# A fifth chunk of q and k split by GpSimd, in the place of the first, with TensorE's order to match

## The reference

```
qn = q / (norm(q, axis=tokens) + 1e-6)      kn = k / (norm(k, axis=tokens) + 1e-6)
a  = softmax(kn.T @ qn / tau)               # 256 x 256
x  = v @ a                                  # 6016 x 256
h  = x @ w_in1;  x = (max(h, 0) ** 2) @ w_out1
h  = x @ w_in2;  y = max(0.01 * h, h) @ w_out2
```

## Time and profile before

| | us |
|---|---|
| median of 3 runs | 1022.01 (1021.99 to 1022.23) |
| the profiled run | 1026.41 |
| span of its records | 1024.6 |
| TensorE busy in the span | 1018.3 (99%) |
| VectorE, ScalarE, GpSimd busy | 726.7, 673.4, 26.4 |
| granted TensorE clock, from 0 to 75 us | 1.00 in each 5 us |

### The profile page before, as it was taken

How to read it: one execution, slowest core, us unless ns; L and a number is a source line. 1 busy time by engine, 2 the same in 40 slices (tenths; PEclk the granted TensorE clock), 3 DMA queues, 4 the chain that set the end, 5 groups by cost and what they waited for, 6 DMA issues and landing times.

```text
span 1024.6 us, 13174 instructions
## 1 busy us (share of the span) xinstructions
PE 1018.3 (99%) x4602; PEld 860.6 (84%) x4602; DVE 726.7 (71%) x1195; ACT 673.4 (66%) x1186; POOL 26.4 (3%) x34
## 2 busy tenths in 40 slices
PE   9999999999999999999999999999999999999998
PEld 8888888888888888888888888888888888888887
DVE  6899867667666667667567767768777777777665
ACT  7788877777777777777666556555655556555554
POOL 3600000000000000000000000000000000000000
PEclk9999999999999999999999999999999999999999
DMA  9711020131131122124452002002002002000001
GB/s 365 264 58 32 20 92 32 67 137 32 67 114 54 67 98 71 46 98 158 144 181 91 1 3 80 1 0 80 1 1 80 1 1 82 1 1 29 12 0 42
DMA packets 33874, 69.27 MB, mean 68 GB/s; under 512 B 2832, under 2 KB 18704, under 8 KB 33808
## 3 DMA queue, kind: packets, MB, share of 16 engines
q1 hardware_dynamic: 33232, 67.25, 18.9%
q10 hardware_dynamic: 576, 1.18, 0.3%
HBM read 44.56 MB, written 23.86 MB: 67 GB/s over the span
## 4 chain that ended last, share of the span: by engine, by line
PE 98%; DMA 0%; DVE 0%; issue 0%; ACT 0%; ACTq 0%; DVEq 0%
PE psum L518 32%; PE psum L520 32%; PE psum L519 32%; PE psum L525 3%; DMA qk<-in_k 0%; DVE q_inv L1086 0%; DVE k_den L1084 0%; PE psum L581 0%; ACT out_buf L997 0%; DVE s_neg L1094 0%; PE psum L570 0%; DVE s_min L1097 0%; ACTq L721 0%; ACT q_norm L809 0%; ACT e L803 0%
## 5 line engine op out<-in xcount | busy, mean ns | idle before, releaser
L860 ACT ACTIVATE g_hi<-g 128x496 fp32r<-128x496 f32 (+1 forms) x384 | 237.3, 618 | 200.3 <-DVE g L1157 76.5
L1147 DVE TENSOR_TENSOR g_lo<-g,g_hi 128x496 fp32r<-128x496 f32 (+1 forms) x384 | 259.7, 677 | 137.5 <-ACT g_hi L860 135.1
L518 PE MATMUL psum<-g_hi,wout_hi 128*128 128x496 f32 (+1 forms) x768 | 295.5, 385 | 0.0
L519 PE MATMUL psum<-g_lo,wout_hi 128*128 128x496 f32 (+1 forms) x768 | 295.4, 385 | 0.0
L520 PE MATMUL psum<-g_hi,wout_lo 128*128 128x496 f32 (+1 forms) x768 | 295.4, 385 | 0.0
L520 PE MATMUL psum<-xop_hi,win_lo 128*128 128x496 f32 (+1 forms) x672 | 258.5, 385 | 0.0
L518 PE MATMUL psum<-xop_hi,win_hi 128*128 128x496 f32 (+1 forms) x672 | 258.5, 385 | 0.0
L519 PE MATMUL psum<-xop_lo,win_hi 128*128 128x496 f32 (+1 forms) x672 | 258.5, 385 | 0.0
L518 PEld LDWEIGHTS psum<-g_hi,wout_hi 128*128 128x128 f32 x768 | 144.2, 188 | 26.7 <-issue 0.3
L519 PEld LDWEIGHTS psum<-g_lo,wout_hi 128*128 128x128 f32 x768 | 144.2, 188 | 26.5
L520 PEld LDWEIGHTS psum<-g_hi,wout_lo 128*128 128x128 f32 x768 | 144.2, 188 | 26.5
(11 more groups left out here) (103 smaller groups left out, 690.4 us busy)
## 6 DMA issues: line engine op xcount, KB each, us to landing
up_parts<-park_up SPq DMA_DIRECT2D x8, 896.0 KB, 4.2
qk<-in_q SPq DMA_DIRECT2D x15, 384.0 KB, 8.1
qk<-in_k SPq DMA_DIRECT2D x13, 384.0 KB, 9.6
stage_o<-in_w_out SPq DMA_DIRECT2D x16, 256.0 KB, 3.4
down_parts<-park_down SPq DMA_DIRECT2D x8, 512.0 KB, 2.8
raw<-in_vT SPq DMA_DIRECT2D x8, 496.0 KB, 4.8
x_tiles<-out_buf SPq DMA_DIRECT2D x8, 496.0 KB, 3.1
raw<-x_tiles SPq DMA_DIRECT2D x8, 496.0 KB, 4.2
```

Of the source, the lines that this page charges most:

```text
L518: pe.matmul(out, a_hi, b_hi, start=start and i == 0, stop=False, **more)
L519: pe.matmul(out, a_hi, b_lo, start=False, stop=False, **more)
L860: act.activation(g_hi[:, tile, 0:W], g[:, tile, 0:W], ACT.Copy).then_inc(g_hi_made[tile], 1)
L1147: dve.tensor_tensor(g_lo[:, tile, 0:W], g[:, tile, 0:W], g_hi[:, tile, 0:W].bitcast(F32), ALU.subtract).then_inc(g_split[tile], 1)
```

## The change

Line 23 to 27, GpSimd's loop and the places of the split chunks. GpSimd now splits chunks 3, 6, 8, 10 and 12. Chunk 5 is no longer split; 3 and 6 are. There are still four places: `SPLIT_PLACES` gives chunk 3 place 2, chunk 6 place 0, chunk 8 place 1, chunk 10 place 3, and chunk 12 place 2 again. Before it splits chunk 12 GpSimd waits until TensorE has used chunk 3. TensorE takes chunk 4 ahead of 3, and 5 and 7 ahead of 6. ScalarE's waits follow the places.

```
-MAIN_CHUNKS = (0, 1, 2, 3, 4, 6, 7, 5, 9, 11, 8, 10)
+MAIN_CHUNKS = (0, 1, 2, 4, 3, 5, 7, 6, 9, 11, 8, 10)
 TAIL_CHUNKS = (13, 14, 12)
-SPLIT_CHUNKS = (5, 8, 10, 12)
+SPLIT_CHUNKS = (3, 6, 8, 10, 12)
+SPLIT_PLACES = (2, 0, 1, 3, 2)
...
         split_places = (o_win_hi + 7168, o_win_lo + 7168, o_wout_hi, o_wout_hi + 12288)
-        qk_hi = [at(f"qk_hi{n}", [P, 2, QK_TILES, C], F32R, o) for n, o in enumerate(split_places)]
-        qk_lo = [at(f"qk_lo{n}", [P, 2, QK_TILES, C], F32R, o + 6144) for n, o in enumerate(split_places)]
+        qk_hi = [at(f"qk_hi{n}", [P, 2, QK_TILES, C], F32R, split_places[s]) for n, s in enumerate(SPLIT_PLACES)]
+        qk_lo = [at(f"qk_lo{n}", [P, 2, QK_TILES, C], F32R, split_places[s] + 6144) for n, s in enumerate(SPLIT_PLACES)]
...
+                if SPLIT_PLACES[n] in SPLIT_PLACES[:n]:
+                    wait_used(pool, SPLIT_CHUNKS[SPLIT_PLACES.index(SPLIT_PLACES[n])])
                 pool.wait_ge(qk_loaded[slot], 32 * (c // QK_SLOTS + 1))
...
-                for c in SPLIT_CHUNKS[0:2]:
-                    wait_used(act, c)
+                for c, place in zip(SPLIT_CHUNKS, SPLIT_PLACES):
+                    if place < 2:
+                        wait_used(act, c)
...
-                    for c in SPLIT_CHUNKS[2:4]:
-                        wait_used(act, c)
+                    for c, place in zip(SPLIT_CHUNKS, SPLIT_PLACES):
+                        if place >= 2:
+                            wait_used(act, c)
```

## The result

The changed kernel takes **1027.01 us** (six runs, 1026.26 to 1028.68), the kernel before 1022.12 (six runs, 1021.96 to 1022.37): a ratio of 1.0049, 95% interval 1.0038 to 1.0059. It is slower by 4.9 us, where 1021.5, 0.5 faster, was forecast, in a range that ended at 1022.8.

The account below looks back on a forecast made before the run. TensorE was taken to bound the kernel (busy 1018.3 of 1024.6 us), waiting only before the transposes of e, where GpSimd sets the chain. q_inv's 0.50 counted, TensorE's 0.19 not added: 1022.01 - 0.50 = 1021.5, range 1020.5 to 1022.8.

Parts of the forecast that it names:

- I carry the difference over: Whole kernel: the profiled run's 4.40 us over the timed median stays, so 1022.01 - 0.50 = 1021.5; chance 0.51.
- the ends of GpSimd's two last operations do: Chain before the transposes of e: T2's and T3's ends set it through q_den and k_den, not q_norm's end at 42.03.
- Now q_den, asking at 41.87, waits for **T1, not T2: VectorE's q_den: done at 42.78 behind T1, with k_den behind T2, so q_inv starts 0.50 us earlier.
- TensorE's part: TensorE's gram matmuls: chunk 3 becomes a split chunk standing alone, gaining 0.165 to 0.215 us, taken as 0.19.
- GpSimd's part: GpSimd's splits: no rest from 18.63, ending at 40.26, 1.46 later; wi_lo then holds T1 until about 41.36.
- wi_lo holds GpSimd: VectorE's first wi_lo: holds T1 until 41.36, costing T1 0.72 us, hidden before ScalarE takes T1 up.
- rival 1: At T1: GpSimd is not held by wi_lo; q_inv starts near 43.35, 1020.8, or near 42.8, 1020.3; chance 0.20.
- k_den done at 44.08: VectorE's k_den: waits for T2, not T3; q_inv starts there instead of at 44.57, 0.50 us earlier.
- Rival 3: At q_inv: it asks for the shared port and waits for T3, 0.7 to 0.8 us more, 1022.7; chance 0.11.
- up to the point where the idle 1.85 us is used up: TensorE before the transposes of e: moving 47.99 moves the end equally until the idle time is gone; 1.54 us left.
- The queues: SyncE's loads: chunk 13 is issued 1.1 us later, with 8.9 left to land, so no delay is taken.
- Rival 4: Whole kernel: over 2 us, slower if GpSimd were delayed beyond chunk 12's cover; chance 0.03 slower, 0.02 faster.

Follow-up runs that it names:

- experiment 1: The kernel before, run and traced again with no edit: 1022.04 us (ten runs); the traced run is the one of 1022.46.
- experiment 7: The kernel before with two warm-up matmuls of TensorE instead of six, to make the late start on purpose: 1025.25 us.
- experiment 8: The kernel before with two warm-up matmuls instead of six and GpSimd's T1 made to wait for q_den and k_den: 1023.42 us.
- experiment 6: The changed kernel with GpSimd's T1 made to wait until q_den and k_den are done: 1023.19 us.
- experiment 3: The changed kernel with VectorE's first wi_lo moved behind the first scores: 1022.43 us, ratio 0.9993 to the kernel before.
- experiment 2: The changed kernel with 12 matmuls on constants before the transposes of e, filling TensorE's idle time: 1025.32 us.
- experiment 4: The changed kernel with four split chunks, 6, 8, 10 and 12 (no chunk 3), and TensorE's order to match: 1026.68 us.
- experiment 5: The changed kernel with chunks 3, 5, 8, 10 and 12 split (5 kept, not 6) and TensorE's order to match: 1024.37 us, in four heaps.

## Why the prediction was wrong, step by step

- **"Span 1024.6 to 1024.1; the profiled run took 1026.41, 4.40 over the median of the timed runs, and I carry the difference over": this is the step that failed.** The 4.40 us were no overhead that both kernels carry. They were a run in which TensorE started late and q_den was caught by T2 and k_den by T3: in experiment 1 neither is caught and the transposes come 3.87 earlier, and experiments 7 and 8 make the late start, and take the wait away from it, on purpose. The run of 1022.46 has neither wait. So "the ends of GpSimd's two last operations do" (set the chain) was right of the trace and wrong of the kernel that is timed, and "Now q_den, asking at 41.87, waits for **T1, not T2**" was counted as a gain of one operation where it was the loss of two: q_den behind T1 and k_den behind T2, worth 2.08 us by experiment 6, before the clock.
- **TensorE's part**, 0.165 to 0.215: mis-sized. From the start of chunk 3 or 4 to the sums over sq_sum it is 24.17 us in experiment 1 (14.98 to 39.15) and 23.72 in the changed kernel (15.02 to 38.74): 0.45. An unsplit chunk ahead of a split one took 2.40 (15.02 to 17.42), less than both bounds. The earlier trace rows had it: four unsplit chunks in a row took 10.18 and two 4.99, so one more costs 2.595, and one alone comes to 2.395. With that the gain is 10.18 less 2.395, 4.99 and 2.33, so 0.465. It changed nothing in the end: the gain came in front of a wait.
- **GpSimd's part** held: a start at chunk 6's landing (18.26), no rest, and wi_lo asking inside the second-last subtraction. The last subtraction went first, the second of the two ways that were given. Its end came at 39.89 and not 40.26: the split of chunk 6 started at 18.26 and not at 18.63. Raw tile 0 came only 0.13 earlier (T1 starts at 40.51).
- **wi_lo holds GpSimd**, the choice between the forecast and rival 1, is right: T1 took 1.61, and T3 2.27 in experiment 3.
- **k_den done at 44.08**: measured 43.49, q_inv from 43.48. Against the trace of before the transposes moved by 1.08 and not by 0.50; the span grew by 0.3 all the same, which leaves 1.4 for the clock once more.
- **Rival 3** is off: q_inv takes 1.74 with T3 beside it, and 1.74 in the trace of before, where T3 was over 0.06 after its start.
- **"up to the point where the idle 1.85 us is used up"**, and the sum's 1.54 us idle: idle time was counted as free. It came out at 3.03 and took 1.4 us more by the clock (experiment 2). No rival priced that.
- **The queues**: chunk 13 is squared at 32.99, no later than before; no split tile was late. Right.
- **Rival 4**, over 2 us slower, was given 0.03, by a mechanism that did not occur. What occurred was a race of q_den against T1's start (40.96 and 40.51); the prediction set q_den (41.87) only against T1's end (41.91), as its trace had q_den behind T1 already. The row to ask for was that of a run of 1022.0 us.

With traces of the right kind on both sides: the transposes come at 44.12 before (experiment 1) and 46.91 after, 2.79 later; to the second transposes it is 4.23 before and 5.67 after, 1.44 more, with the fall of the clock. Together that is 4.23, and the two traced runs are 4.26 apart (1022.46 and 1026.72). The medians are 4.9 apart since one traced run was above its median and the other below.

## What to carry to other kernels

Where a profiled run is slower than the timed ones by more than they vary (here 4.40 against 0.24), find out what is different in it before a sum is made from its rows. Where two engines keep one another out, look at who asks first and how far apart they are: here 0.4 us of room decided over 3 us, and a change that only keeps an engine off the critical path busy 1.2 us longer (39.89 against 38.73) used it up. Idle time of TensorE is free only while its clock stays up.

## What the runs showed of the hardware

- VectorE and GpSimd hold each other off for whole instructions in both directions: q_den, some 0.28 us alone, takes 1.30; T3, 1.27 alone, takes 2.27. This agrees with the Trainium skill (SBUF — State Buffer, "Who interferes with whom"), by which whoever comes first holds the shared pair of ports for the whole instruction and the other is blocked. The reciprocal, which the section does not name, ran beside T3 unhindered (1.74).
- With one of VectorE's instructions waiting, GpSimd's next one, already queued, went first in three traces (wi_lo behind both last subtractions, in the changed kernel and in experiments 4 and 6), while VectorE's q_den went ahead of T2 in the changed kernel and of T3 in the trace of before; T2 had to wait for T1's semaphore, T3 for nothing. Whether that decides who goes first was not tried.
- The granted clock fell to 0.50 after TensorE had stood still for 3.03 and for 2.54 us, and didn't after 1.85, 1.73, 1.62 and 1.27 (before, experiments 7, 5 and 6). The clock came back within 4 us.
- TensorE's plain matmuls took 634 ns a record until 9.6 us in the trace of before, with a granted clock that is listed as 1.00; in experiment 1 all but the first of chunk 0 take 379. That column does not tell the two starts apart, the duration of the records does.
